# Attention and two expert layers on one core: first weights loaded later, sums copied by two engines, GpSimd reordered

## The reference

```
kv  = einsum('bhsd,bhse->bhde', k, v)            # b=4, h=8, s=576, d=64
x   = einsum('bhsd,bhde->bhse', q, kv)
x   = x / sqrt(mean(x*x, -1) + 1e-6) * g_norm    # then (b*s, h*d) = (2304, 512)
h   = x @ w_in1;  x = (h * sigmoid(1.702*h)) @ w_out1     # w_in 512x2048, w_out 2048x512
h   = x @ w_in2;  out = softplus(h) @ w_out2
```

## Time and profile before

| what | value |
|---|---|
| median of three runs | 828.81 us (827.93 to 829.47) |
| profiled execution | 826.74 us |
| its span | 825.0 us |
| TensorE busy | 806.2 us (98%) |
| VectorE busy | 581.5 us (70%) |
| ScalarE busy | 427.0 us (52%) |
| GpSimd busy | 222.6 us (27%) |
| HBM traffic over the span | 168 GB/s |

### The profile page before, as it was taken

The page is one execution under the profiler, slowest core; times in us unless marked ns, Lnnn a source line. Parts: engine busy times, 40 slices in busy tenths (PEclk is TensorE's granted clock), DMA queues, the critical chain, the costliest instruction groups (busy, mean ns, idle before and its releaser), DMA issues.

```text
span 825.0 us, 12369 instructions
## 1 busy us (share of the span) xinstructions
PE 806.2 (98%) x4600; PEld 733.3 (89%) x4600; DVE 581.5 (70%) x1023; ACT 427.0 (52%) x815; POOL 222.6 (27%) x263
## 2 busy tenths in 40 slices
PE   7988999999999999999999999999999999999998
PEld 7877999989999999999998888888898988889886
DVE  3685666696656687675687777888767888666774
ACT  4662233243122143223247777678767678766765
POOL 5987878114133003263521351000000000000000
PEclk9999999999999999999999999999999999999999
DMA  9946346432744642656653537223443422452312
GB/s 357 406 177 250 137 170 255 174 120 90 247 172 169 226 157 90 225 208 256 215 201 108 201 118 272 111 90 134 151 150 102 167 90 91 154 190 90 136 44 76
DMA packets 24426, 139.78 MB, mean 169 GB/s; under 512 B 2224, under 2 KB 6960, under 8 KB 17200
## 3 DMA queue, kind: packets, MB, share of 16 engines
q1 hardware_dynamic: 24224, 138.95, 46.1%
q10 hardware_dynamic: 144, 0.07, 0.0%
HBM read 104.92 MB, written 34.08 MB: 168 GB/s over the span
## 4 chain that ended last, share of the span: by engine, by line
PE 79%; DVE 6%; POOL 5%; ACT 4%; DMA 4%; issue 2%; SPq 0%; ACTq 0%; DVEq 0%; POOLq 0%
PE ps L614 37%; PE ps L675 20%; PE ps L683 14%; PE ps L680 8%; DMA w_in_f<-w_in 2%; POOL w_in L462 2%; DVE gs_f L988 1%; DMA w_out_f<-w_out 1%; POOL xs L495 1%; DVE xs_f L959 1%; ACT ex L787 1%; ACT fix L789 1%; ACT ex L785 1%; DMA kv_in_sb<-k_v 1%; DVE gs_f L1032 1%
## 5 line engine op out<-in xcount | busy, mean ns | idle before, releaser
L614 PE MATMUL ps<-xs,w_in 128*128 128x384 f32 x2016 | 411.0, 339 | 8.7 <-DVE gs_f L988 3.9
L614 PEld LDWEIGHTS ps<-xs,w_in 128*128 128x128 f32 x2016 | 356.7, 188 | 35.7 <-issue 4.4
L675 PE MATMUL ps<-w_out,gs 128*128 128x512 f32 x864 | 226.3, 394 | 1.0 <-issue 0.6
L988 DVE TENSOR_TENSOR gs_f<-ps,gs_f 128x384 f32<-128x384 f32 x240 | 133.4, 556 | 118.2 <-PE ps L614 116.4
L675 PEld LDWEIGHTS ps<-w_out,gs 128*128 128x128 f32 x864 | 160.0, 188 | 25.7 <-issue 1.7
L683 PE MATMUL ps<-gs,w_out 128*128 128x512 f32 x576 | 148.2, 392 | 0.0
L683 PEld LDWEIGHTS ps<-gs,w_out 128*128 128x128 f32 x576 | 105.6, 188 | 16.4
L462 POOL TENSOR_TENSOR w_in<-w_in_f,w_in 128x256 fp32r<-128x256 f32 x112 | 93.3, 870 | 42.3 <-ACT w_in L817 35.6
L779 ACT ACTIVATE lg<-gs_f 128x384 f32<-128x384 f32 x73 | 38.1, 525 | 124.9 <-DVE gs_f L988 124.8
L1040 DVE TENSOR_TENSOR gs<-gs_f,gs 128x384 fp32r<-128x384 f32 x96 | 55.3, 576 | 45.1 <-ACT gs L812 42.5
L680 PE MATMUL ps<-gs,w_out 128*128 128x256 f32 x576 | 84.5, 282 | 0.0
(11 more groups left out here) (65 smaller groups left out, 580.8 us busy)
## 6 DMA issues: line engine op xcount, KB each, us to landing
w_in<-w_kept SPq DMA_DIRECT2D x40, 1792.0 KB, 7.5
w_kept<-w_in SPq DMA_DIRECT2D x16, 1792.0 KB, 11.2
w_in_f<-w_in SPq DMA_DIRECT2D x16, 512.0 KB, 4.1
w_out_f<-w_out SPq DMA_DIRECT2D x16, 512.0 KB, 8.8
kv_in_sb<-k_v SPq DMA_DIRECT2D x8, 640.0 KB, 11.4
kv_in_sb<-k_v SPq DMA_DIRECT2D x8, 576.0 KB, 12.5
q_sb<-q_t SPq DMA_DIRECT2D x16, 288.0 KB, 11.4
out<-xy SPq DMA_DIRECT2D x18, 256.0 KB, 7.8
```

Source lines behind the costliest of these rows:

```text
L614: mm = nc.tensor.matmul(ps[:, bank, 0:HALF], w[:, wp, W_OF[k], cols], xs[:, k, xp, t], start=(new and t == 0 and (wp, xp) == (HI, HI)), st ...
L675: mm = nc.tensor.matmul(ps[:, acc_bank(1, j), 0:DM], g[:, j * P:(j + 1) * P], w, start=new, stop=done)
L988: nc.vector.tensor_tensor(to, bank, other, ALU.add).then_inc(added, 1)
```

## The change

- `W_AT` moves the loads of the first three pairs of weights from behind the queries of units 0, 5 and 8 to behind those of units 4, 8 and 12.
- The sums of the first pair of weights are made by VectorE (`first_w_sums`) behind `scale(4)`; GpSimd waits for them.
- The tails of the keys of two units lie in one tile, each on its own 64 partitions, without zeros; a pair of units takes 18 tiles of 128 columns in `kv_in_sb` where it took 19.
- GpSimd's order up to step 1 is another: the block B11 of x first, then the first weights, B21, the second weights, T3, T2, T4, T1, B22, the second matrix's first pair, and only then sums, rounding and low parts of the third weights. The wait ahead of the last two is for two of the four tiles of step 0's gate, where it was for all four (ahead of the low parts alone).
- VectorE makes T3 and T2 both in unit 9, T4 in unit 10 and T1 in unit 11 (it was one in each of units 9 to 12). In step 0 its last addition (C12_ADD) stands ahead of the gate's product of C21.
- In step 1, ScalarE rounds the weights of pair 3 behind `hidden(m, C22)`, where it did so ahead of `hidden(m, C21)`.
- Both of the last pairs of `w_out` of layer 1 are split in step 6, and none in step 7. `SWAP_AT` loses step 23 and gains step 29.
- Between chunks, VectorE copies two of the six banks of sums (`by_vector`), for the last chunk of layer 1 and the first two of layer 2, behind C12_ADD; ScalarE copies the others, partly in another place.

```diff
-        X_EARLY = (B11, B21, B22, T3, T2, T4, T1)
+        X_EARLY = (B11, B21, T3, T2, T4, T1, B22)
...
-        SWAP_AT = (18, 19, 20, 21, 22, 23, 26, 28)
+        SWAP_AT = (18, 19, 20, 21, 22, 26, 28, 29)
         def w_out_of(m):
             if m < STEPS:
-                return m, 0
-            if m in SWAP_AT:
-                return SWAP_AT.index(m), 1
-            return None
+                return [(p, 0) for p in ((m,) if m < STEPS - 2 else (m, m + 1) if m == STEPS - 2 else ())]
+            return [(SWAP_AT.index(m), 1)] if m in SWAP_AT else []
...
+        def by_vector(ci, i):
+            return CHUNKS - 1 <= ci < 2 * CHUNKS - 1 and i in ((2, 3) if ci < CHUNKS else (0, 1))
...
-            W_AT = {0: 0, 5: 1, 8: 2}
+            W_AT = {4: 0, 8: 1, 12: 2}
...
             nc.gpsimd.memset(sq_sb[:, 1, 0:P], 0.0).then_inc(warm_zeroed, 1)
-            w_sums(0)
+            x_early(B11)
+            pool.wait_ge(w_summed, 4)
             w_high(0)
             w_low(0)
-            x_early(B11)
+            x_early(B21)
             w_sums(1)
-            x_early(B21)
             w_high(1)
             w_low(1)
-            w_sums(2)
-            w_high(2)
             for slot in X_EARLY[2:]:
                 x_early(slot)
-            w_out_low(0)
-            pool.wait_ge(g_split, TILES)
+            w_out_low(0, 0)
+            w_sums(2)
+            pool.wait_ge(g_split, C21 + 1)
+            w_high(2)
             w_low(2)
...
-                if split_at(m):
+                if split_at(m) and m > 1:
                     round_w_in(split_at(m))
...
-                if begins_late:
-                    copy_sums(ci - 1, 0, 1)
-                elif begins:
-                    copy_sums(ci - 1, 0, first_copies(ci - 1))
+                if begins:
+                    copy_sums(ci - 1, 0, KT // 2 if ci < CHUNKS else 1)
                 hidden(m, C22)
-                if begins_late:
-                    copy_sums(ci - 1, 1, 2)
+                if m == 1:
+                    round_w_in(split_at(m))
                 if m >= PHASE1:
                     round_g(m, C21)
+                if begins and ci == CHUNKS:
+                    copy_sums(ci - 1, 1, 2)
+                if begins_late:
+                    copy_sums(ci - 1, 0, ACC_BANKS // 2)
                 hidden(m, C12)
-                if begins_late:
-                    copy_sums(ci - 1, 2, 3)
...
+            def first_w_sums():
+                w32 = w_in32[:, split_buffer(0), LO]
+                dve.wait_ge(w_in_landed[split_buffer(0)], 16)
+                nc.vector.tensor_tensor(w32[:, S3], w32[:, A11], w32[:, A21], ALU.subtract).then_inc(w_summed, 1)
...
                 scale(u)
+                if u == PAIRS:
+                    first_w_sums()
                 if u == 2 * PAIRS + 1:
                     dve.wait_ge(x_made, 2 * PAIRS)
-                if 0 <= u - 2 * PAIRS - 1 < 4:
-                    raw_x(0, X_RAW_ORDER[u - 2 * PAIRS - 1])
+                    raw_x(0, T3)
+                    raw_x(0, T2)
+                if u == 2 * PAIRS + 2:
+                    raw_x(0, T4)
+                if u == 2 * PAIRS + 3:
+                    raw_x(0, T1)
...
                 if m == 0:
                     gate_split(m, C11)
+                    add(m, C12_ADD)
...
+                if p == 0 and ci >= CHUNKS:
+                    copy_sums(ci - 1)
```

More of the change, by code:

```diff
@@ L199, in kv_tile @@
             first = kv_piece(u).start + 2 * t * P
[L200 removed]
+            rows = slice(0, P)
             if t == MAIN:
                 first = 2 * MAIN * P
[L203 removed]
+                rows = slice(TAIL, P) if u % 2 else slice(0, TAIL)
+            return kv_in_sb[rows, slot, first:first + P], kv_in_sb[rows, slot, first + P:first + 2 * P]
         def q_tokens(u, slot):
@@ L339, in acc_bank, with copies, wait_copied, sums_copy @@
             return ACC_BANK + (j if phase == 0 else (j + KT) % ACC_BANKS)
-        def acc_copies(ci):
-            return ACC_BANKS * ci
+        def by_vector(ci, i):
+            return CHUNKS - 1 <= ci < 2 * CHUNKS - 1 and i in ((2, 3) if ci < CHUNKS else (0, 1))
+        def copies(ci, i, vector):
+            return sum(by_vector(c, k) == vector for c in range(ci + 1) for k in range(ACC_BANKS)
+                       if c < ci or k <= i)
+        def wait_copied(engine, ci, i):
+            if by_vector(ci, i):
+                engine.wait_ge(sums_out, copies(ci, i, True))
+            else:
+                engine.wait_ge(acc_copied, copies(ci, i, False))
+        def sums_copy(ci, i):
+            tok = ci % CHUNKS * CHUNK
+            done = tiles_done(STEPS * ci)
+            if ci >= CHUNKS:
+                return done + i + 1, tile_rows(ci, i), ps[:, acc_bank(1, i)].rearrange("p (a n) -> p a n", a=2)
+            if i < KT // 2:
+                return (done + 2 * i + 2, xy[:, 2 * i:2 * i + 2, tok:tok + NARROW],
+                        ps[:, ACC_BANK + KT + i].rearrange("p (a n) -> p a n", a=2))
+            j = i - KT // 2
+            return done + KT + j + 1, xy[:, j, tok + NARROW:tok + CHUNK], ps[:, ACC_BANK + j]
         def tile_rows(ci, j):
@@ L468, in w_high, with w_out_low @@
                 pool.wait_ge(w_hi_early, d + 1)
-            def w_out_low(m):
-                pair, layer = w_out_of(m)
+            def w_out_low(pair, layer):
                 t = w_out_tile(pair)
-                if m == 0:
+                if pair == 0 and layer == 0:
                     pool.wait_ge(w_out_landed[pair], 16)
@@ L521, in _ @@
                     w_sums(d)
-                if w_out_of(m):
-                    w_out_low(m)
+                for pair, layer in w_out_of(m):
+                    w_out_low(pair, layer)
                 if d:
@@ L832, in copy_sums @@
             def copy_sums(ci, first, last):
-                tok = ci % CHUNKS * CHUNK
                 for i in range(first, last):
[L836 to L848, removed]
+                    if not by_vector(ci, i):
+                        done, to, sums = sums_copy(ci, i)
+                        act.wait_ge(acc_tile_done, done)
+                        nc.scalar.copy(to, sums).then_inc(acc_copied, 1)
             def first_copies(ci):
@@ L875, in _ @@
                     hidden(m, C11)
-                if w_out_of(m) and m > 0:
-                    round_w_out(m)
-                if split_at(m):
+                if m > 0:
+                    for pair, layer in w_out_of(m):
+                        round_w_out(pair, layer)
+                if split_at(m) and m > 1:
                     round_w_in(split_at(m))
@@ L996, in _, with copy_sums @@
                 scale(u)
+                if u == PAIRS:
+                    first_w_sums()
                 if u == 2 * PAIRS + 1:
                     dve.wait_ge(x_made, 2 * PAIRS)
-                if 0 <= u - 2 * PAIRS - 1 < 4:
-                    raw_x(0, X_RAW_ORDER[u - 2 * PAIRS - 1])
+                    raw_x(0, T3)
[4 more added lines that the diff above has]
+                    raw_x(0, T1)
+            def copy_sums(ci):
+                for i in range(ACC_BANKS):
+                    if by_vector(ci, i):
+                        done, to, sums = sums_copy(ci, i)
+                        dve.wait_ge(acc_tile_done, done)
+                        nc.vector.tensor_copy(to, sums).then_inc(sums_out, 1)
             def hidden_of(m, tile):
@@ L1103, in _ @@
                         gate_split(m, C21)
-                add(m, C12_ADD)
+                if m > 0:
+                    add(m, C12_ADD)
                 if ends:
```

24 lines of the change are left out of this document (13 added, 11 removed).

## The result

| what | before | changed |
|---|---|---|
| median, 12 runs each in turns | 828.92 us (826.40 to 829.47) | 823.79 us (821.91 to 827.92) |
| ratio changed / before | | 0.9947, 95% interval 0.9930 to 0.9963 |
| profiled execution, span | 826.74, 825.0 us | 825.46, 823.7 us |
| a second set of runs | 828.23 us | 825.25 us (822.28 to 827.40), ratio 0.9965 (0.9952 to 0.9977) |

The change makes the kernel faster, by 3 to 5 us where I had forecast 9.3. The first median lies 0.3 above the range that I gave (816.9 to 823.5), the second 1.75 above it.

The account below looks back on a forecast made before the run. TensorE bounds undisturbed steps (15.73 us), so only waits can be won, with GpSimd's chain deciding the start. Gains of 6.2 up to P1 of step 3, 0.9, 0.8 and 1.4 sum to 9.3: 819.5 us predicted, range 816.9 to 823.5.

Parts of the forecast that it names:

- Late steps: Step 7 gains 0.9 us, step 25 0.8, steps 33 and 41 together 1.4; `SWAP_AT` 0.
- late copies give nothing: Rival, chance 0.06: VectorE, behind in step 24, passes its lateness on; 821.7 us.
- What made P1 of step 2 wait: Steps 1 and 2: C21's sigmoid stood behind ScalarE's rounding of pair 3, late through GpSimd's sums; the 3.62 us wait goes.
- Loads: Attention: 0.85 MB less ahead of unit 10's keys, 2.1 us; product near 29.9, P6 could start at 47.3.
- First sums on VectorE: Attention, behind scale(4): four operations of about 0.42 us, 1.7 in all, ending at 22.8 in VectorE's idle time.
- GpSimd's chain: Deciding term from 22.8 on: T2 ready at 47.9, `down` of step 0 at 60.5, 1.4 us gained, bounds 3.0 and -1.
- behind 62: Sign that the forecast is wrong: `down` of step 0 starts later than 62 us.
- the slower case: Rival, chance 0.03: all GpSimd work at the contended rate, factor 1.37, `down` 12.7 us late; 835 us.
- VectorE's C12_ADD and two raw sums: C12_ADD ahead takes 0.8 off the 1.51 us wait, worth nothing here; raw sums in unit 9 cost 0 to 0.5, hidden.
- Waits and the clock: Steps 1 and 2: waits left are 1 us or less, shorter than the 1.51 followed by a clock of 1.00.
- The stall only moved: Rival, chance 0.16: GpSimd's chain 3 us longer, wait for ScalarE's rounding returns at step 2's end; 823 to 825 us.

Follow-up runs that it names:

- the late edits alone: Kernel before with only the changes from step 6 on (`SWAP_AT`, `w_out` in step 6, sum copies by two engines): 824.74 us, ratio 0.9962.
- the one-edit kernel: Kernel before with one edit: in step 1 ScalarE rounds pair 3's weights behind the sigmoid of C22: 824.17 us, ratio 0.9957.
- the run with the tails alone: Kernel before with only the key tails of a pair of units in one tile: 827.48 us, ratio 0.9989.
- the better profile: Second profile of the unaltered changed kernel, 822.28 us, without the cold first products; its set of runs: 825.25 us, ratio 0.9965.
- the kernel with pair 0 early: Changed kernel with pair 0 loaded behind unit 0 again, its sums, rounding and low parts on GpSimd ahead of B11: 819.99 us, ratio 0.9899.
- the two with late loads and without them: Old loads, tails, raw sums and GpSimd order with the rest of the change: 818.92 us; that with loads at units 4, 7, 10, VectorE first sums, B11 first: 827.83.
- the run with the raw sums spread: Changed kernel with padded key tails and raw sums T3, T2, T4, T1 one in each of units 9 to 12: 824.35 us, ratio 0.9952.
- the old start: Changed kernel with old loads, tails, raw sums and GpSimd order; late edits, ScalarE's order, C12_ADD ahead and two-tile gate wait kept: 818.92 us, ratio 0.9885.
- padded tails: Changed kernel with the old padded key tails, 128 rows each, 64 KB more per pair of units: 823.08 us, ratio 0.9946.

## Why the prediction was wrong, by its own steps

**Late steps: right.** Forecast 0.9 + 0.8 + 1.4 = 3.1; measured 3.2 and 3.4 in the changed kernel, 3.6 with the late edits alone. Step 25 gave less (0.24), as most of its gain fell in step 24, which went from 16.44 to 16.07. The rival "late copies give nothing" is out.

**What made P1 of step 2 wait: right.** ScalarE's rounding ahead of C21's sigmoid was the cause, which the one-edit kernel shows: 4.1 us.

**Loads: earlier, by less than forecast, and worth nothing.** Unit 10's product was forecast for 29.9, 2.1 earlier than before, and came at 30.63, 1.4 earlier. But P6 starts at 49.96, against 49.88 before: it cannot start ahead of GpSimd's T2, ready at 49.91, however early the keys are. That the tails cost TensorE nothing, which the sum took without a reason, was also wrong in the small: 0.15 us for each unit, hidden in the kernel before, as the run with the tails alone shows.

**First sums on VectorE: right.** Four of 0.42, as estimated. They end at 23.08 (forecast 22.8), and GpSimd's cast follows at 23.14.

**GpSimd's chain: this step failed.** I priced it by means of the earlier trace rows and wrote: "The means there show that the two engines meet in a few operations only." Both sets of low parts behind that mean (pair 0's and pair 1's, 4.86 and 4.84) had ended by 34.71, and VectorE's first raw sum started at 37.30; the cast beside it, at 37.65, took 2.29 where the two before took 1.68. The change puts pair 1's set beside the raw sums. Term by term, in the better profile:

| step of the chain | forecast | measured | what was missed |
|---|---|---|---|
| T2 ready | 47.9 | 49.91 | start 0.3; low parts of pair 1 6.87, not 4.85 |
| `w_out` of step 0 ready | 60.5 | 62.87 | 0.4 more on it (cast 1.37) |
| `down` of step 0 | 60.5 | 63.39 | VectorE's gate of C21, 63.29, comes after `w_out` |
| P1 of step 2 | 75.3 | 78.13 | nothing more |
| from `w_out` of step 0 to that of step 1 | 16.1 | 18.9 | two sets of sums 3.94 and 3.97, not 2.9; low parts 5.63, not 5.35; `w_out` 3.4, not 3.0 |
| `down` of step 1 | 76.6 | 81.84 | GpSimd's rows above, 2.4 and 2.8 |
| P1 of step 3 | 91.5 | 96.62 | |

So the terms that were mis-sized are the prices of GpSimd's low parts of pair 1 and of its later sums. The 5.1 us at P1 of step 3 come down GpSimd's chain alone, as it has no pause up to 81.78; VectorE's 0.5 us at the first `down` are hidden behind it. The 5.1 are the whole miss of that profile: 822.28 against the 817.4 that I gave for a profiled execution. The bound that I had set for `down` of step 0 ("behind 62") is the one that was crossed. The contended rate stood in my rows, as 6.66 against 4.85 for the low parts, but I used it only for the slower case, at all operations, and not for those that would now run beside VectorE's work. With 6.8 for pair 1 and 1.0 for each of the eight later sums, 4.1 of the 5.1 would have been in the sum.

**The removed idle time.** I did name that before, GpSimd "did pair 0 while nobody needed it". The change gives that up: 4 sums, a cast and 7 low parts, which run from 8.94 to 18.5 in the kernel with pair 0 early. Sums went to VectorE, but the cast and the low parts (6.53 us) joined a chain that has no pause any more. The kernel with pair 0 alone put back, and the two with late loads and without them, show this from both sides. How much of the loss is the lost idle time and how much the stretched operations was not separated: with pair 0 early, pair 1's low parts still take 6.29 and a set of sums 3.6, but the chain has room for it.

**VectorE's C12_ADD and two raw sums: partly wrong.** I cost the two raw sums in unit 9 at 0 to 0.5. They took 3.1 us together, the root of unit 10 waited on ScalarE for them, and ahead of `kv_sb` stood that root. ScalarE's timeline shows the queue:

```profile
39.87 0.30 ACT L762 ACTIVATE rms<-rms,eps_col 128x8 f32<-128x8 f32 x1 [3.03 <-DVE rms L946]
40.07 0.46 ACT L785 COPY gs_f<-ps 128x384 f32<-128x384 f32 x1
40.43 0.44 ACT L756 COPY kv_sb<-ps 64x64 f32<-64x64 f32 x2
```

That is TensorE's 0.93 at 41.01. It costs little in the end, as T2 sets P6 anyway; the run with the raw sums spread has no such wait and is no faster.

Moving C12_ADD ahead took 0.7 off the wait at P1 of step 1 (1.51 to 0.83), where I had forecast 0.8. I had named the gate of C21 behind it and put no wait to it; it makes `down` of step 0 wait, 1.01 in the changed kernel and 1.00 with pair 0 early. In the old start, where VectorE's gate operations are not stretched, the same order costs 0.13.

**Waits and the clock.** I left waits of 1 us or less without a price. In the first profile, waits of 1.11 and 0.83 stand ahead of this stretch at half clock; with padded tails, 1.12, 0.82 and 1.02 stand ahead of the second row:

```profile
64.40:67.80 3.40, 3.23 (x13) 2.75 (x12) 3.30 (x5) 1.00 (x2) 3.32 (x4) 0.53 1.00 323
```
```profile
63.40:66.80 3.40, 3.40 (x16) 3.40 (x16) 2.30 (x3) 0.00 (x0) 3.26 (x5) 0.53 0.99 415
```

The second profile of the changed kernel has nearly the same waits and no such stretch. So several short waits close together can be enough, in some executions. That is a fall I had ruled out when I took the 1.51 us of the kernel before, with a clock of 1.00 behind it, as the measure. The Trainium skill (TensorE: Matmul & The Clock Gate, the part on the clock gate) says that the count of cold matmuls varies from run to run; the starts of the two profiles agree with it, three key products of 1.53 us in one and none in the other. The fall costs little by itself here: the step that holds it takes 17.77 against 17.04, and the next `down` then waits 1.84 in place of 2.48, since GpSimd is the bound.

**The rivals.** "The stall only moved" gave 823 to 825 with a chance of 0.16, and is the one that happened in amount. Its place was another: not ScalarE's rounding at the end of step 2, but GpSimd's `w_out` at the start of it. The slower case needed 9 us of lateness; it was 2.9 at the first `down` and 5.2 at the second.

**Left open.** The changed kernel's runs spread over 5 to 6 us, while the four of the old start lie within 1.0. The cold start (2.42 between two profiles) and the clock are my reading of it, from profiles of single executions; no run isolates them. The old start had slow first products in its profile too, and still has the narrow spread. Whether the pair of VectorE's additions or the wait for two tiles gives the rest of the old start's lead (about 2 us beyond the sum of late edits and ScalarE's order) was not separated either.

## What to carry to other kernels

An engine that is 27% busy over the span can be the bound in one stretch. Price a chain without pauses by what each operation costs beside the work that will run next to it, and not by a mean from a quieter stretch. Work that sits in an engine's idle time was free here, and a load moved later to help the DMA queue took that away; so ask first what else the loaded data was feeding. Where an instruction waits for two engines, look up when each was done: the row names one of them only. Where one wait has several causes, try the cheapest edit alone: moving one instruction on ScalarE gave 4.1 us, as much as the whole change (3 to 5).

## What was unexpected in the hardware

- GpSimd's and VectorE's operations with two inputs in SBUF take longer when they overlap: GpSimd 6.87 against 4.85 for seven (1.4 times), VectorE 1.77 against 0.96 (768 columns) and 1.58 against 0.55 (384 columns, at 61.45 in the kernel before, with GpSimd idle). Not every overlap does it: the raw sum at 41.04 takes 0.96 beside the same seven low parts. The Trainium skill (SBUF — State Buffer, "Who interferes with whom") says that such an operation of VectorE contends with GpSimd's reads, and that issue order decides who blocks; here both lose, in turn, within the same stretch. VectorE's casts are stretched as well, 0.78 against 0.36 (384 columns), and GpSimd's, 1.57 against 0.83 in the rows above.
- A key product whose tail has 64 rows costs TensorE more and not less than the padded one of 128 rows. In the attention of the changed kernel (mean ns of one behind the busy time; the padded one takes 227 throughout):

```profile
L568 PE MATMUL ps<-kv_in_sb 128*64 128x64 f32 x200 | 8.6, 227 | 1.4 <-ACT kv_sb L756 0.9 <-DMA kv_in_sb<-k_v 0.5
L568 PE MATMUL ps<-kv_in_sb 64*64 64x64 f32 x48 | 4.0, 242 | 0.0
```

- When TensorE speeds up at the start varies between executions of the same kernel: key products of 1.53 us up to 11.50 in one, 0.95 from 5.45 on in another, while the granted clock of both reads 1.00.
